# First group of heads and first layer pairs: other order on TensorE, ScalarE and VectorE, first weight tile last in the DMA queues, rests in pieces

## The reference

```python
# q, k, v: (4, 8, 576, 64); x: 2304 tokens x 512
kv = np.einsum('bhsd,bhse->bhde', k, v)
out = np.einsum('bhsd,bhde->bhse', q, kv)
rms = np.sqrt(np.mean(out * out, axis=-1, keepdims=True) + 1e-06)
attn = out / rms * g_norm                                   # -> x, (2304, 512)
h = x @ w_in;  g = h * (1.0 / (1.0 + np.exp(-h)));  x = g @ w_out     # d_ff 2048
a = x @ w_a;   b = x @ w_b;                         y = (a * b) @ w_out2   # d_ff 1536
```

## Time and profile before

| what | value |
|---|---|
| median of three runs | 906.86 us |
| the profiled execution | 905.95 us |
| its span in the trace | 903.9 us |
| TensorE busy | 864.6 us (96%) |
| VectorE, ScalarE, GpSimd busy | 512.1, 285.5, 618.5 us |
| granted TensorE clock | full in all 40 slices |

### The profile page before, as it was taken

The page is one execution under the profiler, slowest core; times in us unless marked ns, Lnnn a source line. Parts: engine busy times, 40 slices in busy tenths (PEclk is TensorE's granted clock), DMA queues, the critical chain, the costliest instruction groups (busy, mean ns, idle before and its releaser), DMA issues.

```text
span 903.9 us, 16943 instructions
## 1 busy us (share of the span) xinstructions
PE 864.6 (96%) x6564; PEld 817.2 (90%) x6564; DVE 512.1 (57%) x816; ACT 285.5 (32%) x479; POOL 618.5 (68%) x869
## 2 busy tenths in 40 slices
PE   5797989999999999999999999999999999999998
PEld 4697889998899999999989999999998999999996
DVE  2575465546886656565683553562565544545535
ACT  2683444434443222223441221221242212211210
POOL 1786445563687677775578787977979877777760
PEclk9999999999999999999999999999999999999999
DMA  9841312411011111111101111111210250111103
GB/s 259 206 95 56 81 47 59 114 36 37 24 47 48 47 47 48 47 30 42 47 25 47 47 47 48 47 47 33 62 48 23 67 155 25 48 48 47 47 24 105
DMA packets 38782, 55.62 MB, mean 62 GB/s; under 512 B 2608, under 2 KB 23088, under 8 KB 38704
## 3 DMA queue, kind: packets, MB, share of 16 engines
q1 hardware_dynamic: 35984, 49.55, 19.5%
q10 hardware_dynamic: 2720, 4.98, 1.9%
HBM read 49.81 MB, written 4.72 MB: 60 GB/s over the span
## 4 chain that ended last, share of the span: by engine, by line
PE 84%; DVE 8%; POOL 3%; ACT 2%; issue 2%; DMA 1%; SPq 0%; ACTq 0%; POOLq 0%; DVEq 0%
PE ps L709 43%; PE ps L773 7%; PE ps L774 6%; PE ps L775 6%; PE ps L795 5%; PE ps L797 5%; PE ps L796 5%; PE ps L666 2%; PE ps L725 1%; PE ps L676 1%; DVE g_lo L1340 1%; DVE xy L1354 1%; PE ps L641 1%; DMA kvq<-in_q_dram 1%; PE ps L654 1%
## 5 line engine op out<-in xcount | busy, mean ns | idle before, releaser
L709 PE MATMUL ps<-x_hi,w_hi 128*128 128x288 f32 x1092 | 236.7, 298 | 3.9 <-ACT kept L1024 2.5
L709 PE MATMUL ps<-x_lo,w_hi 128*128 128x288 f32 x1092 | 234.0, 296 | 0.0
L709 PE MATMUL ps<-x_hi,w_lo 128*128 128x288 f32 x1092 | 232.9, 295 | 0.0
L709 PEld LDWEIGHTS ps<-x_hi,w_hi 128*128 128x128 f32 x1092 | 179.0, 188 | 16.7 <-issue 6.4
L709 PEld LDWEIGHTS ps<-x_hi,w_lo 128*128 128x128 f32 x1092 | 176.1, 189 | 0.0
L709 PEld LDWEIGHTS ps<-x_lo,w_hi 128*128 128x128 f32 x1092 | 174.8, 188 | 0.0
L448 POOL TENSOR_SCALAR w_hi<-wt 128x256 fp32r<-128x256 f32 x156 | 69.6, 446 | 140.5 <-PE ps L709 136.3
L773 PE MATMUL ps<-g_hi,d_hi 128*128 128x288 f32 x512 | 154.5, 302 | 8.7 <-DVE xy L1354 5.5
L1024 ACT COPY kept<-ps 128x576 f32<-128x576 f32 x117 | 75.3, 643 | 241.8 <-PE ps L709 241.3
L774 PE MATMUL ps<-g_lo,d_hi 128*128 128x288 f32 x512 | 150.9, 295 | 0.0
L775 PE MATMUL ps<-g_hi,d_lo 128*128 128x288 f32 x512 | 150.8, 295 | 0.0
(11 more groups left out here) (101 smaller groups left out, 1186.7 us busy)
## 6 DMA issues: line engine op xcount, KB each, us to landing
raw<-in_moe_w_out_dram SPq DMA_DIRECT2D x28, 512.0 KB, 3.8
raw<-in_moe_w_in_dram SPq DMA_DIRECT2D x15, 512.0 KB, 3.8
raw<-in_moe_w_a_dram SPq DMA_DIRECT2D x12, 512.0 KB, 3.6
raw<-in_moe_w_b_dram SPq DMA_DIRECT2D x12, 512.0 KB, 3.5
kvq<-in_k_dram SPq DMA_DIRECT2D x12, 288.0 KB, 5.4
kvq<-in_v_dram SPq DMA_DIRECT2D x12, 288.0 KB, 7.0
kvq<-in_q_dram SPq DMA_DIRECT2D x12, 288.0 KB, 8.6
out_dram<-xy SPq DMA_DIRECT2D x27, 128.0 KB, 2.4
```

What stands on the lines that cost most here:

```text
L709: mm = pe.matmul(ps[:, bank + s, 0:PART], w, x[:, n, c, s * PART:(s + 1) * PART], start=(begins and first), stop=last, skip_group_check=no ...
```

## The change

It makes six edits.

1. The transfers of the first weight tile (`raw_half`) are issued behind the heads of all four head pairs, on SP and on ACT, where they stood behind the third.
2. In group 0, `kv(0, 2)` and `kv(0, 3)` run behind the `q_turn`s of the pair before, where each stood inside the head pair before its own; their evictions stand behind `root`. `half_round(6, 0)` moves from in front of the last `root` to behind `kv_keep(1, 0)`, with `half_round(6, 1)`; the rounds and rests of operand 3 come before those of 6.
3. On DVE in the second pair, flushes stand ahead of the rests of operand 4 and of `silu`; the norm of group 1 is spread over three slots.
4. On DVE in every layer-1 pair, flushes 10 and 11, 12 and 13, 14 and 15 stand together; before, the second of each two stood behind the next `silu` or `g_rest`. The sums `x_half` are spread as well.
5. POOL's `x_rest` is issued as four instructions of 128x288 where it was one of 128x1152; the sum `x_sum_of(1, 5)` is made a pair earlier.
6. `last_round` on ACT stands behind the three `part`s.

```diff
-    FIRST_ROUNDS = (..., (3, 0), (6, 0), (3, 1), (6, 1), (5,), (1,), (2,), (4,))
+    FIRST_ROUNDS = (..., (3, 0), (3, 1), (6, 0), (6, 1), (5,), (1,), (2,), (4,))
@@ SP, heads of group 0 (the same on ACT with raw_half(1))
-                if h == 2:
-                    sp.dma_start(*raw_half(0)).then_inc(raw_in[0], 16)
+            sp.dma_start(*raw_half(0)).then_inc(raw_in[0], 16)
@@ POOL x_rest
-                nc.gpsimd.tensor_tensor(x_lo[:, n], operand(seg, n), x_hi[:, n].bitcast(F32),
-                                        ALU.subtract).then_inc(side_ready, 1)
+                for c in range(2):
+                    for part in (slice(0, PART), slice(PART, SEQ)):
+                        op = nc.gpsimd.tensor_tensor(x_lo[:, n, c, part], operand(seg, n)[:, c, part],
+                                                     x_hi[:, n, c, part].bitcast(F32), ALU.subtract)
+                op.then_inc(side_ready, 1)
...
-                if pp == 5:
+                if pp == 4:
                     pool.wait_ge(x_kept, UNITS + UNITS // 2)
                     x_sum_of(1, 5)
@@ PE, group 0
-                    if j == 1 and h + 1 < PAIRS:
-                        kv(0, h + 1)
+                    if h == 0 and j == 1:
+                        kv(0, 1)
                 if h + 1 < PAIRS:
                     for j in range(JS):
                         q_turn(0, h + 1, j, j)
+                if h + 2 < PAIRS:
+                    kv(0, h + 2)
@@ ACT first_pair
                 half_round(3, 1)
+                attend(0, True)
+                half_round(6, 0)
                 half_round(6, 1)
-                attend(0, True)
@@ ACT layer1 (last_round moves likewise in layer2)
-                last_round(pp)
                 next_round(pp, 0)
...
                 part(u, 2)
                 attend(at + 2, False)
+                last_round(pp)
@@ ACT, group 0
-                    if j == 1 and h + 1 < PAIRS:
-                        kv_keep(0, h + 1)
+                    if h == 0 and j == 1:
+                        kv_keep(0, 1)
                 if h == 3:
                     half_round(3, 0)
-                    half_round(6, 0)
                 root(0, h)
+                if h + 2 < PAIRS:
+                    kv_keep(0, h + 2)
@@ DVE norm(at)
-                if at < STEPS * PAIR0[1] and h < PAIRS and a == 8:
-                    invert(1, h)
-                    for j in range(JS):
-                        normalise(1, h, j)
+                if at < STEPS * PAIR0[1] and h < PAIRS and 8 <= a <= 10:
+                    if a == 8:
+                        invert(1, h)
+                    normalise(1, h, a - 8)
@@ DVE first_pair: the rests of operand 4 move from its end into second_pair
@@ DVE layer1, second half (before, then after)
-                add(u, 1, halves(held[:, 2, :]))
-                g_rest(pp, 1)
-                flush(12)
-                silu(pp, 2)
-                norm(at + 5)
-                attend(at + 6)
-                flush(13)
-                next_rest(pp, 2)
-                add(u, 2, both(BANK_C))
-                flush(14)
-                g_rest(pp, 2)
-                flush(15)
-                silu(pp, 3)
-                norm(at + 6)
-                g_rest(pp, 3)
-                if pp in (5, 6):
-                    x_half(pp - 5)
+                add(u, 1, halves(held[:, 2, :]))
+                flush(12, 13)
+                g_rest(pp, 1)
+                silu(pp, 2)
+                norm(at + 6)
+                attend(at + 6)
+                next_rest(pp, 2)
+                add(u, 2, both(BANK_C))
+                flush(14, 15)
+                g_rest(pp, 2)
+                silu(pp, 3)
+                g_rest(pp, 3)
+                if pp in (5, 6):
+                    x_half(1, pp - 5)
```

More of the change, by code:

```diff
@@ L1275, in half_rest, with x_half @@
                                         ALU.subtract).then_inc(x_ready, 1)
-            def x_half(c):
+            def x_half(n, c):
                 s1, s2, s4, s3 = temps(1)
@@ L1281, in x_half @@
                     dve.wait_ge(qT_mm, 2 * UNITS)
-                    dve.wait_ge(side_sum, x_summed(1, 5)[1])
                 dve.wait_ge(x_kept, UNITS + JS * (3 + c))
-                nc.vector.tensor_tensor(s2[:, c], quad(1, 1, 1)[:, c], s3[:, c], ALU.subtract).then_inc(x_sum, 1)
-                nc.vector.tensor_tensor(s1[:, c], quad(1, 1, 0)[:, c], quad(1, 1, 1)[:, c], ALU.add).then_inc(x_sum, 1)
-                dve.wait_ge(x_sum, 3 + 3 * c + 1)
-                nc.vector.tensor_tensor(s4[:, c], quad(1, 0, 1)[:, c], s2[:, c], ALU.subtract).then_inc(x_sum, 1)
+                if n == 1:
+                    dve.wait_ge(*x_summed(1, 5))
+                if n == 4:
+                    dve.wait_ge(x_sum, 3 + 3 * c + 1)
+                dst, a, b, op = {1: (s2, quad(1, 1, 1), s3, ALU.subtract), 4: (s4, quad(1, 0, 1), s2, ALU.subtract),
+                                 2: (s1, quad(1, 1, 0), quad(1, 1, 1), ALU.add)}[n]
+                nc.vector.tensor_tensor(dst[:, c], a[:, c], b[:, c], op).then_inc(x_sum, 1)
             def x_rest(seg, n):
@@ L1367, in first_pair @@
                 half_rest(3, 0)
+                half_rest(3, 1)
                 half_rest(6, 0)
-                half_rest(3, 1)
+                half_sum(1)
                 half_rest(6, 1)
-                half_sum(1)
                 half_sum(2)
@@ L1388, in first_pair @@
                 attend(6)
-                half_rest(4, 0)
-                half_rest(4, 1)
             def second_pair():
@@ L1398, in flush @@
                         flush1(0, n)
-                flush(0, 4)
+                flush(0, 1)
                 norm(at + 1)
+                flush(2, 4)
+                norm(at + 2)
+                half_rest(4, 0)
                 flush(5, 7)
+                norm(at + 3)
+                half_rest(4, 1)
                 add(u, 0, both(BANK_B))
-                flush(8, 9)
+                flush(8, 11)
                 silu(1, 0)
-                flush(10, 11)
                 g_rest(1, 0)
+                flush(12, 13)
                 add(u, 1, halves(held[:, 2, :]))
                 silu(1, 1)
-                flush(12, 12)
                 g_rest(1, 1)
-                flush(13, 13)
                 silu(1, 2)
                 add(u, 2, both(BANK_C))
-                flush(14, 14)
+                flush(14, 15)
                 g_rest(1, 2)
-                flush(15, 15)
                 silu(1, 3)
@@ L1422, in layer1, with flush @@
                 u, at = prods_of(pp)[0], STEPS * pp
-                def flush(n):
-                    flush1(pp - 1, n)
+                def flush(first, last):
+                    for n in range(first, last + 1):
+                        flush1(pp - 1, n)
+                norm(at)
                 attend(at)
-                flush(0)
-                flush(1)
-                norm(at)
+                flush(0, 1)
                 late_rest(pp, 0)
+                if pp == 7:
+                    x_half(2, 1)
@@ L1432, in layer1 @@
+                norm(at + 1)
                 attend(at + 1)
-                flush(2)
-                flush(3)
-                flush(4)
-                norm(at + 1)
+                flush(2, 4)
                 late_rest(pp, 1)
                 next_rest(pp, 0)
+                if pp in (6, 7):
+                    x_half(*((2, 0), (4, 1))[pp - 6])
+                norm(at + 2)
                 attend(at + 2)
-                flush(5)
-                flush(6)
-                flush(7)
-                norm(at + 2)
+                flush(5, 7)
@@ L1444, in layer1 @@
                 next_rest(pp, 1)
+                if pp == 6:
+                    x_half(4, 0)
+                norm(at + 3)
                 attend(at + 3)
                 add(u, 0, both(BANK_B))
-                flush(8)
-                flush(9)
+                flush(8, 9)
                 silu(pp, 0)
-                norm(at + 3)
+                norm(at + 4)
                 attend(at + 4)
                 g_rest(pp, 0)
-                flush(10)
+                flush(10, 11)
                 silu(pp, 1)
-                flush(11)
@@ L1456, in layer1 @@
-                norm(at + 4)
+                norm(at + 5)
                 attend(at + 5)
                 add(u, 1, halves(held[:, 2, :]))
+                flush(12, 13)
                 g_rest(pp, 1)
-                flush(12)
                 silu(pp, 2)
-                norm(at + 5)
+                norm(at + 6)
                 attend(at + 6)
-                flush(13)
                 next_rest(pp, 2)
                 add(u, 2, both(BANK_C))
-                flush(14)
+                flush(14, 15)
```

7 lines of the change are left out of this document (3 added, 4 removed).

## The result

The changed kernel takes 916.45 us, the median of four runs (916.02 to 916.89), against 906.91 us of the kernel before beside it (905.19 to 907.5). The ratio is 1.0108, with a 95% interval of 1.0091 to 1.0126: 9.5 us slower. The prediction was 899.0 us, faster. It had the wrong sign.

The account below looks back on a forecast made before the run. The prediction took PE, busy 96% of the span, to bound the kernel, leaving 39.3 us idle; its terms summed to -7.8 us, from 905.95 to 898.1, stated as 899.0 with 0.9 for the median, range 896.5 to 901.5.

Parts of the forecast that it names:

- Each ordinary layer-1 pair: Ordinary layer-1 pairs: flush 15 ahead delays part 0 by 0.42 us against 0.27 slack; 1.1 us lost, bounds 0 and 3.
- slower by the paired flushes: Rival: flush 15 delays part 0 by a full tile and flush at 14 layer-1 boundaries; 911.3 us, chance 0.04.
- given back: Rival: gains in the attention pairs are lost again to ACT's chain; 904.5 us, from 901.5 to 905, chance 0.22.
- 97 to 262 us: Stretch from 97 to 262 us: PE's waits on norm and flushes shrink; 4.4 us gained, bounds 2 and 6.3.
- Group 0: Group 0: kv waits for transfers and the late tile delays POOL; 0.8 us slower, between 2.8 faster and 3.5 slower.
- Pair 0: Pair 0: later rounds of operand 6 make PE wait 0.9 us more on g_rest(0, 0), bounds 0 and 1.2.
- The order of 3 and 6 on DVE: Pair 0: new order of operands 3 and 6 on DVE costs nothing, or 0.5 us if the cover goes.
- Second pair: Second pair: earlier flushes and spread norm remove PE's waits; 4.8 us gained of 6.0 idle, bounds 3 and 5.6.
- no wait over 0.6: Sign in the second pair that would show the forecast right: PE has no wait longer than 0.6 us.
- Changes of segment: Two changes of segment: POOL's pieces let DVE in sooner; 0.9 us gained twice, 1.8, bounds 0 and 4.3.
- Segment 3: Segment 3: four POOL pieces take longer than one instruction and delay a weight load; 0.4 us lost, bounds 0 and 1.

Follow-up runs that it names:

- e2: Changed kernel with POOL's sums of activations issued as four instructions of 128x288 instead of one of 128x1152; 903.81 us.
- e6: Changed kernel with flush 15 alone put back behind the third part's rest on DVE, from the ninth layer-1 pair on; 903.99 us.
- e7: Kernel before with flush 15 alone put ahead of the third part's rest on DVE, from the ninth pair on; 920.52 us.
- e9: e6 plus the early sum of segment 1 in four pieces and POOL's rest in one instruction in segment 3 alone; 900.18 us.
- e1: Changed kernel with DVE's order of before in the layer-1 pairs from the ninth on; 904.3 us.
- e5: Changed kernel with POOL's sums in four pieces and POOL's rest in one instruction again at every change of segment; 904.75 us.
- e12: e10 with keys and values of the next head pair made in the pair before its own again, first weight tile still last; 898.61 us.
- e13: e10 with the first weight tile's transfers behind the third head pair again, kv still two pairs on; 899.71 us.
- e10: e9 with rounds and rests of operands 3 and 6 in the order of before on ACT and DVE; 898.26 us.
- e3: Changed kernel with the first weight tile's transfers behind the third head pair again, kv still two pairs on; 918.79 us.
- e4: Changed kernel with rounds and rests of operands 3 and 6 in the order of before on ACT and DVE; 916.76 us.
- e11: e10 with kv in the pair before its own and the first weight tile behind the third head pair, as before; 896.61 us.

## Why the prediction was wrong

**"Each ordinary layer-1 pair", the term of +1.1 us: measured +11.8, and this is the step that failed.** The prediction followed flush 15 as a delay of 0.42 us to `silu`, `g_round` and part 0, and compared it with a slack of 0.27. The delay was sized about right: e2, which keeps the order but has no collision, loses 1.4 us in these pairs for the 1.1 foretold. What was missed stood in the trace beside the earlier trace rows: POOL's sum, 0.08 us behind the rest, in pairs 10 to 13. Four waits of 1.81 us are 7.2 us; two of them (374.34 and 401.91) are followed by 0.66 and 0.57 of granted clock, worth about 1.5 us each (part 0 moves 3.5 us behind the one and 2.0 in a pair without a fall). With the 1.4 us of the delay itself that makes 11.6 of the 11.8. The rival "slower by the paired flushes" had the place and the sign, but another mechanism (a full tile's delay in 14 boundaries), and got 0.04.

**The same collision at the start of pair 4, costed at nothing: +2.0 us.** The changed kernel makes the sum `x_sum_of(1, 5)` there, a pair earlier than before:

```profile
155.58 2.65 POOL L570 TENSOR_TENSOR held<-xy 128x1152 f32<-128x1152 f32 x1
```

```profile
156.29 2.56 DVE L1348 TENSOR_TENSOR g_lo<-held,g_hi 128x576 fp32r<-128x576 f32 x1
```

```profile
161.10 0.37 PE L776 MATMUL ps<-g_hi,d_hi 128*128 128x288 f32 x1 [1.84 <-DVE g_lo L1348]
```

The prediction asked whether POOL had time for the sum, not what DVE does meanwhile. But the move of the sum is not what the trace points at. In the kernel before, with the sum in its old place, the rest had the same lead of 0.08 us over it (DVE and POOL):

```profile
183.98 0.75 DVE L1340 TENSOR_TENSOR g_lo<-held,g_hi 128x576 fp32r<-128x576 f32 x1
184.06 3.20 POOL L571 TENSOR_TENSOR held<-xy 128x1152 f32<-128x1152 f32 x1
```

In the changed kernel flush 15 stands ahead of the rest in pairs 2 to 7 too. In the old place of the sum POOL would have been free for it at 185.6 us and the rest starts at 186.16, so it would have collided there as well. No run moves flush 15 or the sum alone in these pairs (e6 and e7 begin with the ninth, e2 and e9 cut the sum in pieces), so this is argued and not shown.

**Both terms missed the same thing, and the prediction had it in hand.** In the earlier trace rows a DVE instruction starts 0.23 us after POOL's rest and lasts 3.06 us: by this row the one that starts first keeps the port. The prediction used that for the change of segment alone, and wrote that who gets the port next isn't said. The Trainium skill ("SBUF — State Buffer", "SBUF: two separate sides") does say that whichever starts first has the pair for the whole instruction; e6 and e7 agree, 0.75 us with a lead of 0.08 and 2.56 us without. Outside DVE's two-port modes the Trainium skill restricts it there to DVE instructions with two SBUF inputs against a POOL instruction that reads SBUF; the rows agree here as well, since `g_lo<-ps,g_hi`, with one input in SBUF, took 0.74 us beside POOL's `d_lo<-raw,d_hi` (59.46 in e9).

**The other terms were too hopeful by 5 us, which the collision hid.** With it taken out of the ordinary pairs (e1, e2 and e6) the kernel takes 903.8 to 904.3 us, outside the forecast of 896.5 to 901.5. That is in the range of the rival "given back", which had 3.5 for the second pair and 2 for 97 to 262 us, but nothing for the changes of segment. Term by term in the profiled execution of e2: group 0 +0.9 (foretold +0.8), pair 0 +0.9 (+0.9), second pair -2.7 (-4.8), from pair 2 to 7 -2.4 (-4.4), first change of segment -1.6 (-0.9), ordinary pairs +1.4 (+1.1), second change -0.7 (-0.9), segment 3 +2.5 (+0.4); in sum -1.6 (-7.8).

**Group 0, +0.8 us: most of its steps stand, and the size is in the noise.** PE in the changed kernel, answering to the earlier trace rows:

```profile
22.61 1.35 PE L644 MATMUL ps<-kvq 64*64 64x64 f32 x72 [2.06 <-DMA kvq<-in_v_dram]
...
36.53 1.45 PE L657 MATMUL ps<-ident,kvq 128*128 128x128 f32 x9 [0.99 <-POOL kvq L561]
...
38.50 0.55 PE L679 MATMUL ps<-ident,o_sb 128*128 128x128 f32 x3 [0.51 <-DVE o_sb L1239]
```

The kv waits for its transfer until 22.6 and the third `o_turn` comes at 38.50 (38.9 was predicted). The second comes at 31.62 instead of 30.2, behind a fall of the granted clock (0.71 at 22 to 26 us). The stall of 1.33 us called issue at 39.86 is gone whole, where only some of it was counted, so pair 0 begins at 42.35, 0.3 us earlier than before. The executions of e1, e2, e5, e6 and e9, with the same group 0, begin it from 1.2 us earlier to 2.3 later. e12 and e13 fit the reading that kv early only trades one wait for another.

**Pair 0, +0.9 us: +4.9 in the profiled execution, but +0.9 in others.** The late round of operand 6 was foreseen, and its wait is there alone in e1, e2 and e5, which have the same group 0 and pair 0. PE in e1:

```profile
58.84 0.53 PE L728 MATMUL ps<-x_hi,w_hi 128*128 128x288 f32 x2 [0.83 <-DVE g_lo L1348]
```

In the changed kernel, in e6 and in e9 PE waits 1.05 to 1.07 and 2.16 to 2.17 us instead. There DVE's rests and sums of operands 3 and 6, with both inputs in SBUF, fall beside POOL's copies and rests (1.98 us for the rest at 52.63, where e1 has 0.75 at 53.48), and in two of the three the clock falls behind the second wait (0.65 at 60 to 64 us; 1.00 in e6). In these three group 0 had ended 0.1 to 1.2 us earlier than before, in the other three 0.9 to 2.3 later; that this decides it was not tried. The order of 3 and 6 on DVE, costed at nothing or 0.5, is part of it. Putting the old rounds and rests back is worth 1.9 us (e10 against e9).

**Second pair, -4.8: too much, 2.3 to 3.1 in most runs.** That the changed kernel has -4.2 is luck: pair 0 ends 4.6 us late there, and part of the gain only makes that good (e9 is the same, 4.6 and -4.2). Where pair 0 ends 0.6 to 3.1 us late, the second pair gains 2.6 to 2.7 us in e1, e2, e3, e4, e5, e10 and e13, 2.3 in e6 and 3.0 to 3.1 in e11 and e12, at or under the bound of 3. Missed was a wait of PE that is there in each of these runs, where the sign was no wait over 0.6. In the changed kernel:

```profile
93.51 0.51 PE L712 MATMUL ps<-x_hi,w_hi 128*128 128x288 f32 x2 [1.30 <-DVE held L1320]
```

**97 to 262 us, -4.4: in its bounds only without pair 4,** 2.5 without and 0.5 with it; the wait at 127.78, still 1.49 us, is the one of which only a part was counted. **Changes of segment, -1.8: about right,** 1.6 + 0.6, and without the pieces (e5) 0.4 + 0.1. **Segment 3, +0.4:** +0.8 where the clock stays, 2.5 where it falls (e2). The pieces were costed at 0.4 us over one instruction; beside DVE's work they take 4.23 us for 2.68, 1.5 over.

What is left of the change without the collisions and with group 0 as before (e11) is 896.6 us, 9.9 under the kernel before: the gains in the second pair, from 97 to 262 us and at the changes of segment are real, though the first two are smaller than foretold. Where the 1.6 us between e10 and e11 come from stays open.

## What to carry to other kernels

For every DVE instruction that an edit moves or only delays, and that reads and writes only SBUF, look up what POOL starts in the same microsecond, before and after the move, and likewise for every POOL instruction that is moved. A slack of a tenth of a microsecond between two starts can be worth 1.8 us a time, and it stands in no list of waits, because a started instruction that is held counts as busy: look for an instruction that lasts three times its usual time. Where DVE can't be kept ahead, cut POOL's long instruction in pieces, but only there, since the pieces are longer in sum.

## What the runs showed of the hardware

- The first to start keeps its time, and a lead of 0.08 us is enough: DVE first by that, 0.75 us and POOL 3.20; POOL first by 0.73, POOL 2.67 and DVE 2.56 (e6, e7). The cost is not the same for both: 0.5 us for POOL, 1.8 us for DVE.
- Between pieces DVE gets in: beside four POOL instructions of 288 columns (3.68 us in all) DVE's rest took its 0.75 us (e2).
- Waits of PE of 1.8 to 2.2 us were followed by a granted clock of 0.57 to 0.66 in the next 4 us in some cases (374, 402 and 60 us in the changed kernel, 684 us in e1), and by 1.00 in others with the same wait (322 and 348 us; 161 us, where e3, e4 and e6 fall to 0.57; the wait of 2.17 us in pair 0 of e6). What tells them apart was not tried. It makes a wait of 1.8 us cost 2.0 or 3.5, and so two executions of the same orders can differ by some us at one place.
